# Reordering the lead of a fused attention and feed-forward kernel, with the first unit's variance and the next coarse scores each a slot later

## The chip, the cores and the metric

One core of a Trainium2 chip runs the whole program. The metric is the device time in microseconds. The kernel before took 765.53 us, the median of three runs (765.14 to 766.44). Engine names: PE is TensorE, DVE is VectorE, ACT is ScalarE, POOL is GpSimd, SP is the engine that issues the DMAs.

## The reference

Three layers in a row, over q, k, v of shape (4, 8, 576, 64), batch, heads, positions, head size, all in float32:

```python
# 1. attention: a coarse part on means over 4 positions, and a local part with |i-j| < 4
out_up    = repeat(softmax(q_d @ k_d.T / 8) @ v_d, 4)
out_local = softmax(where(|i-j| < 4, q @ k.T / 8, -1e9)) @ v
x = (out_up + out_local) laid out as (4, 576, 512)
# 2. layer norm and a feed-forward layer, 512 -> 2048 -> 512, with a residual
xn = (x - mean(x)) / sqrt(var(x) + 1e-6) * g_ln
x = x + relu(xn @ w_ch1) @ w_ch2
# 3. token shift, a squared-relu feed-forward layer 512 -> 1024 -> 512 and a gate
xk = mu_k*x + (1-mu_k)*x_prev;  xr = mu_r*x + (1-mu_r)*x_prev
out = sigmoid(xr @ w_r) * (relu(xk @ w_k)**2 @ w_v)
```

## The kernel before

The 2304 rows are cut into 8 units of 288. Attention of a unit is cut again into 3 windows of 96 rows (n = 0, 1, 2) for the local part, and into 2 halves of the heads for the coarse part. Each of the large products is three matmuls, since each float32 operand is split into a "hi" part, rounded to fp32r, and a "lo" part, the rest; ACT makes the hi parts and DVE or POOL the lo parts.

**The lead.** Unit 0's attention comes first, with nothing beside it. Its steps are `Tk`/`Tq` (turn k and q on PE), `Sd`/`S` (coarse and local scores), `PdT`/`PT` (turn the probabilities), `OD`/`AV` (coarse and local values) and `M` (mean for the layer norm). They are listed in `FIRST` (line 66) with the PSUM pair that each uses, and written out by hand in every engine's program (PE: from line 1170 on). `keep_on` (line 938) issues matmuls whose result nobody reads. PE then waits for the centred x of unit 0 (`x_lo`) and starts the feed-forward.

**The blocks.** The feed-forward of layer 2 is a loop over `m` from 0 to 127 (`M_ALL`), 16 blocks for a unit. In block m, PE issues `up_b(m)` (12 matmuls of 288 columns into psH), `attend(2m)`, `down_b(m-1)` (12 matmuls into psY) and `attend(2m+1)`. ACT makes `h_hi(m)` from psH, DVE makes `h_lo(m)`, and `down_b(m)` waits for it (`h_split`).

**The slots.** `attend(slot)` issues the attention steps of the next unit whose slot it is. `LATER` (line 75) gives the slots, 2 for each block; for unit 1 `BEHIND` = 2 is added. So the coarse scores `Sd(1,0)` stand in slot 4, and `S(1,0)` and `Sd(1,1)` in slot 7. `OWN_FIRST` sets the slot of unit 0's variance `V(0)`: 2. What the other engines do for a step follows at a lag from the step's slot: in `ACT_WORK` the exponentials `exp_d` of `Sd` have lag 1; in `DVE_WORK` the maximum `top_d` of `Sd` lag 0 and the sum `sum_d` lag 2; in `POOL_WORK` `norm_d` lag 2, and for `V` `rstd` lag 1. SP stores and loads rstd 3 and 10 slots behind `V`.

**The PSUM pair of the later steps.** All steps of units 1 to 7 use pair 0 (psA). Before a step writes it, `wait_bank_out` (line 450 on) waits until the step before it on that pair has been read out. `S(1,0)` comes next on the pair after `Sd(1,0)`; for an `Sd` the wait is

```python
            elif kind == "Sd":
                eng.wait_ge(d_exped, 2 * u + n + 1)
```

and `d_exped` is raised by the last exponential of `exp_d`. `Sd(1,1)` shares the bank pair with `S(1,0)` and waits for nothing of this kind.

**Order on ACT in a block of unit 0.** It is the order of the text: `h_hi(m)`; then the hi parts of the pieces of w_ch1 that `W1_M` (line 177) gives for block m; then the hi part of one piece of w_ch2, `("w2", (m+1)//4, m+1)`; then `attend(2m)`; `attend(2m+1)`. So block 3 makes the piece `("w2", 1, 4)`, the first of the second quarter of w_ch2, and waits for its load:

```python
                elif name == "w2":
                    act.wait_ge(w2_in[j], 16)
```

**Order on DVE in a block of unit 0.** `h_lo(m)`, `attend(2m)`, the lo parts of the w_ch1 pieces by `W1_M`, `attend(2m+1)`. The weights' quarters are loaded by SP in a fixed order; `load_w2(1)`, the second quarter of w_ch2, is issued behind w_ch1's four. PE's `up_b(4)` needs all four pieces (1, 0) to (1, 3) of w_ch1.

Of the kernel before, what the change touches and what calls it, by code (L numbers as in the profile page):

```python
# [21 lines left out]
def fused_kernel(nc, q, k, v, g_ln, w_ch1, w_ch2, mu_k, mu_r, w_k, w_v, w_r, od_scr, x2_scr, out):  # L22
# [38 lines left out]
    def first_key(w, b):  # L61
# [3 lines left out]

    FIRST = [("Tk", 0, 0, 0), ("Tq", 0, 0, 1), ("G", 0, 0, 3), ("S", 0, 0, 2), ("Tk", 0, 1, 3), ("Tq", 0, 1, 0), ("Tk", 0, 2, 1),
# [3 lines left out]
    N_FIRST = len(FIRST)  # L70

    SLOTS = 2 * NF1
# [12 lines left out]

    OWN = [(0, "V", 0)]

    OWN_FIRST = [(2, "V", 0)]

    ROOT_OUT, ROOT_IN = 3, 10  # L90
    BEHIND = 2
# [3 lines left out]
    KEEP = 256  # L95
# [2 lines left out]

    later = []
    for u in range(1, NU):  # L100
        later += [(SLOTS * (u - 1) + s + (BEHIND if u == 1 else 0), kind, u, n) for s, kind, n in LATER]
    for u in range(NU):
        later += [(SLOTS * u + s, kind, u, n) for s, kind, n in (OWN if u else OWN_FIRST)]
    later.sort(key=lambda x: x[0])
# [65 lines left out]
    for b in range(1, B):  # L170
        behind = BEHIND if b == 1 else 0
        for g, (s, load) in enumerate(((16 + behind, 8), (22, 17 + behind), (28 + behind, 21 + behind), (39, 31))):
# [1 line left out]
            V_LOAD[SLOTS * (2 * b - 2) + load] = (b, g)  # L174


    W1_M = {0: [(1, 0)], 1: [(1, 1)], 2: [(1, 2), (1, 3)], 3: [(2, 0)], 4: [(2, 1)], 5: [(2, 2)],
            6: [(2, 3)], 7: [(3, 0)], 8: [(3, 1)], 9: [(3, 2)], 10: [(3, 3)]}
    M_ALL = NU * NF1
    M_LAST = M_ALL - NF1  # L180
# [14 lines left out]
    with ExitStack() as ctx:  # L195
# [65 lines left out]
        kT = sb(ctx, "kT", [P, KT, S])  # L261
# [9 lines left out]
        ident = sb(ctx, "ident", [P, P])  # L271
# [623 lines left out]
        def _(pe):  # L895
# [29 lines left out]
            def turn_d(u, n):  # L925
                i = place_of["PdT", u, n]
                pe.wait_ge(d_normed, 2 * u + n + 1)
                wait_bank_out(pe, i)
                p = coarse(prob_slot("Sd", u, n), u, n)
                for par in range(2):  # L930
                    for j in range(2):
                        for kh in range(2):
                            at = (2 * j + kh) * GU
                            ins = nc.tensor.transpose(pairs[pair_at(i)][0:GU, par, at:at + GU], p[:, par, j, kh * GU:(kh + 1) * GU],  # L934
                                                      ident[0:GU, 0:GU])
                ins.then_inc(pdt_done, 1)

            def keep_on(n, pair):

                for _ in range(n):  # L940
                    mm(pairs[pair][:, 1, 0:KEEP], ident[:], kT[:, 0, 0:KEEP], start=True, stop=True, skip_group_check=True)

            def add_values():
                for half in range(2):
# [7 lines left out]
            def values_d(u, n):  # L952
                i = place_of["OD", u, n]

                pe.wait_ge(vd_made, 4 * (u // 2) + 2)
                if u == 0 and n == 1:
                    pe.wait_ge(vd_first, 1)
                pe.wait_ge(pdt_out, 2 * u + parts_of("OD", u, n)[-1] + 1)
                wait_bank_out(pe, i)
                for part in parts_of("OD", u, n):  # L960
                    pt = turned_place("PdT", u, part)
                    for j in range(2):
                        for par in range(2):
                            for kh in range(2):
                                at = par * 4 * GU + (2 * j + kh) * GU
                                ins = mm(pairs[pair_at(i)][D * par:D * par + D, 0, (2 * part + j) * GU:(2 * part + j + 1) * GU],  # L966
                                         vd[0:GU, kh, 2 * (2 * part + j) + par, :], pt[0:GU, at:at + GU],
                                         start=(kh == 0), stop=(kh == 1), skip_group_check=True)
                ins.then_inc(od_done, 1)
# [24 lines left out]
            def turn_p(u, n):  # L994
                i = place_of["PT", u, n]
                w = NW_U * u + n
                pe.wait_ge(normed, w + 1)
                wait_bank_out(pe, i)
                p = prob_slot("S", u, n)[0:ROWS]
                for j in range(KT):  # L1000
                    ins = nc.tensor.transpose(turned_bank(i)[:, j * ROWS:(j + 1) * ROWS],  # L1001
                                              p[:, 2 * j * RB:2 * j * RB + RB + KB], ident[0:ROWS, 0:ROWS])
                ins.then_inc(pt_done, 1)

            def values(u, n):
                i = place_of["AV", u, n]
                for part in parts_of("AV", u, n):
                    pe.wait_ge(pt_out, NW_U * u + part + 1)
                    wait_vw(pe, NW_U * u + part)
                wait_bank_out(pe, i)  # L1010
                for part in parts_of("AV", u, n):
                    vw = vw_slot(NW_U * u + part)
                    pt = turned_place("PT", u, part)
                    place = local_place("AV", u, part, BQ)
                    for j in range(KT):
                        for par in range(2):
                            for bl in range(BLOCKS):
                                row = RB * (par ^ bl)
                                keys = slice(row, row + KB)
                                at = j * ROWS + bl * RB  # L1020
                                ins = mm(place[D * par:D * par + D, bl, j], vw[keys, bl, j, :], pt[keys, at:at + BQ],  # L1021
                                         start=True, stop=True, skip_group_check=True)
                ins.then_inc(av_done, 1)
# [160 lines left out]
            add_values()  # L1184
            turn_d(0, 0)
            pe.wait_ge(masked, NW_U)
            keep_on(1, 3)
            turn_d(0, 1)
            values(0, 0)
            pe.wait_ge(vd_first, 1)  # L1190
            keep_on(1, 2)
            turn_p(0, 1)
            values_d(0, 0)
            values_d(0, 1)
            turn_p(0, 2)
            keep_on(1, 2)
            values(0, 1)
            values(0, 2)
            pe.wait_ge(consts, 7)
            keep_on(1, 2)  # L1200
            mean_first(0)
            keep_on(1, 2)
            mean_first(1)
            keep_on(1, 2)
            mean_first(2)
            keep_on(5, 2)
            for slot in range(-LEAD, 0):
                attend(slot)
            for m in range(M_ALL):
# [21 lines left out]
        def _(act):  # L1231
# [54 lines left out]
            def od_o(u, n):  # L1286
                i = place_of["OD", u, n]
                first, last = parts_of("OD", u, n)[0], parts_of("OD", u, n)[-1]
                act.wait_ge(od_done, count_of("OD", u, n))
                if u:  # L1290

                    act.wait_ge(av_done, count_of("AV", u, 0))
                if u >= 1:
                    act.wait_ge(x_made, NW_U * u)
                src = pairs[pair_at(i)][:, 0, 2 * first * GU:2 * (last + 1) * GU]

                nc.scalar.activation(odT[:, 2 * first:2 * (last + 1), :], src.rearrange("p (j g) -> p j g", g=GU), ACT.Copy,
                                     scale=1.0 / FACTOR).then_inc(od_out, 1)
# [140 lines left out]
            pdt_o(0, 1)  # L1439
            pt_o(0, 1)  # L1440
            od_o(0, 0)
            od_o(0, 1)
            pt_o(0, 2)
            hi_weight("w1", 0, 0)
            hi_weight("w1", 0, 1)
            hi_x_first(0)
# [43 lines left out]
        def _(dve):  # L1490
# [264 lines left out]
            for m in range(M_ALL):  # L1755
                u, f = divmod(m, NF1)
                dve.wait_ge(h_hi_ready, m + 1)
                nc.vector.scalar_tensor_tensor(out=h_lo[:, m % 2], in0=psH[:, m % 2, 0:N], scalar=0.0, in1=h_hi[:, m % 2].bitcast(F32),  # L1758
                                               op0=ALU.max, op1=ALU.subtract).then_inc(h_split, 1)
                if m == 0:  # L1760
                    for i in range(HALF):
                        flip("q", 1, 0, i)
                attend(2 * m)
                if m == 1:
                    for i in range(HALF):
                        sum_flipped("q", 1, 0, i)
                if u == 0:
                    for x_ in W1_M.get(f, []):
                        lo_weight("w1", *x_)
                if u == NU - 1:  # L1770
                    if f == 1:
                        dve.wait_ge(av_done, count_by("AV", NU))
                        dve.wait_ge(pt_out, NWIN)
                        nc.vector.memset(x_sh[:, 0, :, 0:1], 0.0).then_inc(lead_zero, 1)
                    if f - 1 in EARLY:
                        lo_mix(0, EARLY[f - 1])
                    if f in EARLY:
                        mix_part(0, EARLY[f])
                    for i in c_weights(f):
                        lo_weight(*c_pieces[i])  # L1780
                if f == 0 and u >= 1:
                    scale_y(u - 1)
                attend(2 * m + 1)
            def lo_k(c, f):
                n = tiles[c][1]
                m = c * NF2 + f
# [64 lines left out]
```

## Time and profile before

| what | value |
|---|---|
| median of 3 runs | 765.53 us |
| the profiled execution | 765.75 us |
| its span | 763.6 us |
| PE busy | 750.5 us, 98% |
| DVE, ACT, POOL busy | 431.5, 272.6, 232.5 us |
| PE in 0 to 10 us | 4.74 us busy |
| PE in 30 to 40 us | 7.86 us busy |
| PE in 50 to 60 us | 10.00 us busy |

The span is the time from the first to the last instruction in the trace; the execution's own time is 2.15 us longer. A timeline row gives the start, the duration, the engine, the line, the output and the inputs, and in brackets how long the engine was idle before it and what ended the idle time. Rows of equal instructions are merged ("x12").

### The profile page before, as it was taken

To read this page: it belongs to the slowest core of one execution; us is meant where nothing else is said; L and a number is where in the kernel's file an instruction comes from. 1 tells how busy PE (TensorE), PEld (TensorE's weight loads), DVE (VectorE), ACT (ScalarE), POOL (GpSimd) and SP (SyncE) were. 2 spreads that over 40 slices of the span, in tenths; PEclk is the share of its full clock that TensorE was granted. 3 is DMA by queue.
4 is the path that set the end of the run, shared out by engine and by line. 5 is a ranking of instruction groups with operands and counts; after the bars stand their busy time and mean duration, and the time that the engine had idled before them with its cause. 6 is when DMAs were issued, how large, how long until landed. Compare 5 with 4: busy or idle time off the path is not lost.

```text
span 763.6 us, 15851 instructions
## 1 busy us (share of the span) xinstructions
PE 750.5 (98%) x6455; PEld 691.8 (91%) x6455; DVE 431.5 (57%) x805; ACT 272.6 (36%) x620; POOL 232.5 (30%) x268
## 2 busy tenths in 40 slices
PE   6899999999999999999999999999999999999998
PEld 5789999999999999999999999998888888888886
DVE  5686863444644354554354332657686776766655
ACT  3854432323223123233223231546334334333322
POOL 4667753132443233345224222004111111111101
PEclk9999999999999999999999999999999999999999
DMA  9894441120450021341011004612003010010010
GB/s 182 209 310 74 93 105 21 27 75 19 86 117 9 16 54 56 71 93 40 14 26 40 15 2 155 215 56 87 0 2 109 1 56 28 1 55 1 1 55 28
DMA packets 116543, 49.67 MB, mean 65 GB/s; under 512 B 95084, under 2 KB 105592, under 8 KB 116472
## 3 DMA queue, kind: packets, MB, share of 16 engines
q1 hardware_dynamic: 116472, 48.68, 25.2%
q8 instruction: 51, 0.84, 0.5%
q14 instruction: 20, 0.16, 0.1%
HBM read 39.20 MB, written 9.45 MB: 64 GB/s over the span
## 4 chain that ended last, share of the span: by engine, by line
PE 94%; SPq 4%; DVE 1%; issue 0%; DMA 0%; ACT 0%; DVEq 0%; ACTq 0%
PE psH L1093 27%; PE psY L1110 27%; PE psH L1144 13%; PE psY L1165 13%; PE psA L1126 6%; PE psA L990 2%; PE psA L1021 2%; SPq L620 1%; PE psA L921 1%; SPq L601 1%; PE psA L966 1%; PE psA L1001 1%; PE psA L934 1%; SPq L589 1%; SPq L624 0%
## 5 line engine op out<-in xcount | busy, mean ns | idle before, releaser
L1093 PE MATMUL psH<-xc_hi,w_hi 128*128 128x288 f32 x512 | 155.0, 303 | 0.5 <-DVE xc_lo L1617 0.5
L1110 PE MATMUL psY<-h_hi,w_hi 128*128 128x288 f32 x512 | 153.0, 299 | 0.0
L1093 PE MATMUL psH<-xc_lo,w_hi 128*128 128x288 f32 x512 | 151.1, 295 | 0.0
L1093 PE MATMUL psH<-xc_hi,w_lo 128*128 128x288 f32 x512 | 151.0, 295 | 0.0
L1110 PE MATMUL psY<-h_lo,w_hi 128*128 128x288 f32 x512 | 150.7, 294 | 0.0
L1110 PE MATMUL psY<-h_hi,w_lo 128*128 128x288 f32 x512 | 150.7, 294 | 0.0
L1758 DVE SCALAR_TENSOR_TENSOR h_lo<-psH,h_hi 128x288 fp32r<-128x288 f32 x128 | 58.3, 456 | 163.3 <-ACT h_hi L1458 162.9
L1458 ACT ACTIVATE h_hi<-psH 128x288 fp32r<-128x288 f32 x128 | 52.4, 410 | 244.4 <-PE psH L1093 243.8
L890 POOL TENSOR_TENSOR relu_k<-relu_k 128x512 f32<-128x512 f32 (+1 forms) x39 | 38.6, 991 | 243.7 <-ACT relu_k L1413 243.7
L1093 PEld LDWEIGHTS psH<-xc_hi,w_hi 128*128 128x128 f32 x512 | 96.1, 188 | 3.5 <-issue 2.2
L1110 PEld LDWEIGHTS psY<-h_hi,w_hi 128*128 128x128 f32 x512 | 96.0, 188 | 1.7 <-issue 1.3
L1093 PEld LDWEIGHTS psH<-xc_hi,w_lo 128*128 128x128 f32 x512 | 96.3, 188 | 0.0
L1110 PEld LDWEIGHTS psY<-h_lo,w_hi 128*128 128x128 f32 x512 | 96.1, 188 | 0.1
L1093 PEld LDWEIGHTS psH<-xc_lo,w_hi 128*128 128x128 f32 x512 | 96.2, 188 | 0.0
L1110 PEld LDWEIGHTS psY<-h_hi,w_lo 128*128 128x128 f32 x512 | 96.0, 188 | 0.0
L1717 DVE RECIPROCAL gate<-gate 128x256 f32<-128x256 f32 x36 | 63.1, 1754 | 1.2
L1165 PE MATMUL psY<-w_hi,kh_hi 128*128 128x512 f32 x144 | 56.3, 391 | 0.2 <-DVE kh_lo L1795 0.2
L1165 PE MATMUL psY<-w_lo,kh_hi 128*128 128x512 f32 x144 | 56.1, 390 | 0.0
L1165 PE MATMUL psY<-w_hi,kh_lo 128*128 128x512 f32 x144 | 56.1, 389 | 0.0
L1413 ACT ACTIVATE relu_k<-psH 128x512 f32<-128x512 f32 (+2 forms) x41 | 22.2, 544 | 59.4 <-PE psH L1144 59.4
L1700 DVE SCALAR_TENSOR_TENSOR mixin<-x_sh,params,mixin 128x512 f32<-128x512 f32 (+1 forms) x40 | 34.8, 871 | 14.5 <-ACT mixin L1383 13.2
L829 POOL TENSOR_TENSOR x<-x,y_tmp 128x288 f32<-128x288 f32 x32 | 25.7, 833 | 48.5 <-DVE y_tmp L1664 48.5
(191 smaller groups left out, 1347.2 us busy)
## 6 DMA issues: line engine op xcount, KB each, us to landing
w_raw<-in_moe_w_ch_dram SPq DMA_DIRECT2D x8, 1024.0 KB, 8.6
v_win<-in_v_dram SPq DMA_DIRECT2D x84, 56.0 KB
x_scratch<-x SPq DMA_DIRECT2D x8, 576.0 KB, 4.5
out_dram<-gate SPq DMA_DIRECT2D x17, 256.0 KB, 2.1
raw<-in_q_dram SPq DMA_DIRECT2D x112, 36.0 KB, 2.1
raw<-in_k_dram SPq DMA_DIRECT2D x96, 36.0 KB, 2.0
v_raw<-in_v_dram SPq DMA_DIRECT2D x12, 288.0 KB
x_sh<-x_scratch SPq DMA_DIRECT2D x3, 1026.0 KB, 5.7
```

Source lines behind the costliest of these rows:

```text
L829: nc.gpsimd.tensor_tensor(x[:, u % 2, d], x[:, u % 2, d], y_tmp[:, d % 2], ALU.add).then_inc(x2_made, 1)
L890: nc.gpsimd.tensor_tensor(r, r, r, ALU.mult).then_inc(k_square, 1)
L1093: ins = mm(psH[:, m % 2, 0:N], ws[a][:, kt, f * P:(f + 1) * P], xx[bb][:, kt], start=(kt == 0 and i == 0), stop=(kt == KT - 1 and i == 2))
L1110: ins = mm(psY[:, d, 0:N], ws[a][:, f, d * P:(d + 1) * P], hs[bb][:, m % 2], start=(f == 0 and i == 0), stop=(f == NF1 - 1 and i == 2))
L1126: ins = mm(psA[:, u % 2, :], xx[a][:, kt, t * P:(t + 1) * P], ws[bb][:, kt, :], start=(kt == 0 and i == 0), stop=(kt == KT - 1 and i == 2))
L1144: ins = mm(psH[:, m % 2, 0:n], ws[a][:, kt, f * P:(f + 1) * P], xx[bb][:, kt, 0:n], start=(kt == 0 and i == 0), stop=(kt == KT - 1 and i = ...
L1165: ins = mm(psY[:, t, :], hs[a][:, m % 2, t * P:(t + 1) * P], ws[bb][:, f, :], start=(f == 0 and i == 0), stop=(f == NF2 - 1 and i == 2))
L1413: nc.scalar.activation(relu_k[:, m % 2, at], psH[:, m % 2, at], ACT.Relu).then_inc(k_relu, 1)
L1458: nc.scalar.activation(h_hi[:, m % 2], psH[:, m % 2, 0:N], ACT.Relu).then_inc(h_hi_ready, 1)
L1700: nc.vector.scalar_tensor_tensor(out=y, in0=x_sh[:, c % 2, kt, 1:n + 1], scalar=(muk_col, mur_col)[which][:, kt:kt + 1], in1=y, op0=ALU.mu ...
L1717: chain(nc.vector.reciprocal(g, g))
L1758: nc.vector.scalar_tensor_tensor(out=h_lo[:, m % 2], in0=psH[:, m % 2, 0:N], scalar=0.0, in1=h_hi[:, m % 2].bitcast(F32), op0=ALU.max, op1 ...
```

## The change

- `FIRST` and PE's hand-written lead: `turn_p(0, 1)` comes ahead of `values(0, 0)`, `turn_p(0, 2)` ahead of `values_d(0, 1)`. `keep_on` takes the columns of one matmul, and stands at other places: 10 of 256 columns and one of 128, where there were 11 of 256. ACT's copies follow the new order: `pt_o(0, 2)` ahead of `od_o(0, 1)`.
- `OWN_FIRST`: `V(0)` goes from slot 2 to slot 3, from ahead of `down_b(0)` to behind it.
- `Sd(1, 0)` goes from slot 4 to slot 5, from ahead of `down_b(1)` to behind it, and all its work on ACT, DVE and POOL goes one slot on with it.
- `W1_M`: the pieces of the second quarter of w_ch1 are made in blocks 1, 2, 2, 3 in place of 0, 1, 2, 2, on ACT (hi) and on DVE (lo), and the order of the weights' semaphore counts follows.
- DVE in block 1: `attend(3)` comes ahead of `sum_flipped("q", 1, 0, i)`.

```diff
--- before.py
+++ after.py
@@ -65,7 +65,7 @@
 
     FIRST = [("Tk", 0, 0, 0), ("Tq", 0, 0, 1), ("G", 0, 0, 3), ("S", 0, 0, 2), ("Tk", 0, 1, 3), ("Tq", 0, 1, 0), ("Tk", 0, 2, 1),
              ("S", 0, 1, 2), ("S", 0, 2, 3), ("Sd", 0, 0, 0), ("Sd", 0, 1, 1), ("PT", 0, 0, 2), ("PdT", 0, 0, 0), ("PdT", 0, 1, 1),
-             ("AV", 0, 0, 3), ("PT", 0, 1, 2), ("OD", 0, 0, 0), ("OD", 0, 1, 1), ("PT", 0, 2, 2), ("AV", 0, 1, 0), ("AV", 0, 2, 1),
+             ("PT", 0, 1, 2), ("AV", 0, 0, 3), ("OD", 0, 0, 0), ("PT", 0, 2, 2), ("OD", 0, 1, 1), ("AV", 0, 1, 0), ("AV", 0, 2, 1),
              ("M", 0, 0, 2), ("M", 0, 1, 3), ("M", 0, 2, 0)]
     N_FIRST = len(FIRST)
 
@@ -85,7 +85,7 @@
 
     OWN = [(0, "V", 0)]
 
-    OWN_FIRST = [(2, "V", 0)]
+    OWN_FIRST = [(3, "V", 0)]
 
     ROOT_OUT, ROOT_IN = 3, 10
     BEHIND = 2
@@ -98,7 +98,7 @@
 
     later = []
     for u in range(1, NU):
-        later += [(SLOTS * (u - 1) + s + (BEHIND if u == 1 else 0), kind, u, n) for s, kind, n in LATER]
+        later += [(SLOTS * (u - 1) + s + (BEHIND + int((kind, n) == ("Sd", 0)) if u == 1 else 0), kind, u, n) for s, kind, n in LATER]
     for u in range(NU):
         later += [(SLOTS * u + s, kind, u, n) for s, kind, n in (OWN if u else OWN_FIRST)]
     later.sort(key=lambda x: x[0])
@@ -174,7 +174,7 @@
             V_LOAD[SLOTS * (2 * b - 2) + load] = (b, g)
 
 
-    W1_M = {0: [(1, 0)], 1: [(1, 1)], 2: [(1, 2), (1, 3)], 3: [(2, 0)], 4: [(2, 1)], 5: [(2, 2)],
+    W1_M = {1: [(1, 0)], 2: [(1, 1), (1, 2)], 3: [(1, 3), (2, 0)], 4: [(2, 1)], 5: [(2, 2)],
             6: [(2, 3)], 7: [(3, 0)], 8: [(3, 1)], 9: [(3, 2)], 10: [(3, 3)]}
     M_ALL = NU * NF1
     M_LAST = M_ALL - NF1
@@ -937,8 +937,7 @@
 
             def keep_on(n, pair):
 
-                for _ in range(n):
-                    mm(pairs[pair][:, 1, 0:KEEP], ident[:], kT[:, 0, 0:KEEP], start=True, stop=True, skip_group_check=True)
+                mm(pairs[pair][:, 1, 0:n], ident[:], kT[:, 0, 0:n], start=True, stop=True, skip_group_check=True)
 
             def add_values():
                 for half in range(2):
@@ -1184,26 +1183,28 @@
             add_values()
             turn_d(0, 0)
             pe.wait_ge(masked, NW_U)
-            keep_on(1, 3)
+            keep_on(KEEP, 3)
             turn_d(0, 1)
+            pe.wait_ge(vd_first, 1)
+            keep_on(KEEP, 2)
+            turn_p(0, 1)
             values(0, 0)
-            pe.wait_ge(vd_first, 1)
-            keep_on(1, 2)
-            turn_p(0, 1)
             values_d(0, 0)
+            keep_on(KEEP // 2, 2)
+            turn_p(0, 2)
             values_d(0, 1)
-            turn_p(0, 2)
-            keep_on(1, 2)
             values(0, 1)
+            keep_on(KEEP, 2)
             values(0, 2)
             pe.wait_ge(consts, 7)
-            keep_on(1, 2)
+            keep_on(KEEP, 2)
             mean_first(0)
-            keep_on(1, 2)
+            keep_on(KEEP, 2)
             mean_first(1)
-            keep_on(1, 2)
+            keep_on(KEEP, 2)
             mean_first(2)
-            keep_on(5, 2)
+            for _ in range(4):
+                keep_on(KEEP, 2)
             for slot in range(-LEAD, 0):
                 attend(slot)
             for m in range(M_ALL):
@@ -1439,8 +1440,8 @@
             pdt_o(0, 1)
             pt_o(0, 1)
             od_o(0, 0)
+            pt_o(0, 2)
             od_o(0, 1)
-            pt_o(0, 2)
             hi_weight("w1", 0, 0)
             hi_weight("w1", 0, 1)
             hi_x_first(0)
@@ -1762,6 +1763,7 @@
                         flip("q", 1, 0, i)
                 attend(2 * m)
                 if m == 1:
+                    attend(2 * m + 1)
                     for i in range(HALF):
                         sum_flipped("q", 1, 0, i)
                 if u == 0:
@@ -1780,7 +1782,8 @@
                         lo_weight(*c_pieces[i])
                 if f == 0 and u >= 1:
                     scale_y(u - 1)
-                attend(2 * m + 1)
+                if m != 1:
+                    attend(2 * m + 1)
             def lo_k(c, f):
                 n = tiles[c][1]
                 m = c * NF2 + f
```

## Rows read from the trace of the kernel before

**Rows 1.** The page's first part: busy time, share of the span, instructions.
```profile
PE 750.5 (98%) x6455; PEld 691.8 (91%) x6455; DVE 431.5 (57%) x805; ACT 272.6 (36%) x620; POOL 232.5 (30%) x268
```
**Rows 2.** Waits of PE: line, releaser, total us, times, longest us.
```profile
PE psA L905 <- POOL masks L770: 4.8, 1, 4.8
PE psA L1050 <- POOL xs L818: 1.4, 1, 1.4
...
PE psA L921 <- DVE qdT L1500: 0.5, 1, 0.5
```
**Rows 3.** Chain of waits, 0 to 100 us: start, us, what.
```profile
44.30 1.80 PE psY L1110 x12
46.11 1.60 PE psH L1093 x12
47.70 1.58 PE psY L1110 x12
```
**Rows 4.** Timeline of PE around blocks 1 to 5.
```profile
39.16 0.72 PE L1050 MATMUL psA<-xs,ones 128*128 128x288 f32 x2 [1.45 <-POOL xs L818]
...
43.59 0.71 PE L921 MATMUL psA<-kdT,qdT 64*72 64x144 f32 x8 [0.55 <-DVE qdT L1500]
...
49.22 0.68 PE L990 MATMUL psA<-kT,qT 64*64 64x56 f32 x32
49.83 0.71 PE L921 MATMUL psA<-kdT,qdT 64*72 64x144 f32 x8
50.47 0.40 PE L1093 MATMUL psH<-xc_hi,w_hi 128*128 128x288 f32 x1
...
55.49 0.67 PE L934 MATMUL psA<-ident,prob 72*72 72x72 f32 x8
```
**Rows 5.** Timeline of ACT in blocks 2 to 4.
```profile
45.45 0.38 ACT L1255 ACTIVATE prob<-psA,bias_d 72x144 f32<-72x144 f32 x1 [0.23 <-DVE bias_d L1531]
...
46.80 0.20 ACT L1255 ACTIVATION_READ_ACCUMULATOR prob<-psA,bias_d 72x1 f32 x1
47.74 0.41 ACT L1458 ACTIVATE h_hi<-psH 128x288 fp32r<-128x288 f32 x1 [0.74 <-PE psH L1093]
48.05 0.72 ACT L1338 ACTIVATE w_hi<-w_raw,params 128x512 fp32r<-128x512 f32 x1
51.60 0.62 ACT L1352 CAST w_hi<-w_raw 128x512 fp32r<-128x512 f32 x1 [2.83 <-DMA w_raw<-in_moe_w_ch_dram]
52.38 0.41 ACT L1458 ACTIVATE h_hi<-psH 128x288 fp32r<-128x288 f32 x1 [0.16 <-PE psH L1093]
...
53.30 0.61 ACT L1352 CAST w_hi<-w_raw 128x512 fp32r<-128x512 f32 x1
53.80 0.37 ACT L1255 ACTIVATE prob<-psA,bias_d 72x144 f32<-72x144 f32 x1
```
**Rows 6.** The DMA issues, timeline of SP.
```profile
39.04 0.65 SPq L624 DMA_DIRECT2D w_raw<-in_moe_w_ch_dram  x1
...
42.13 3.05 SPq L633 DMA_DIRECT2D w_raw<-in_moe_w_ch_dram  x3
```
**Rows 7.** DMA view of 38 to 52 us: mean rate of the window.
```profile
DMA packets 3836, 4.36 MB, mean 312 GB/s; under 512 B 1937, under 2 KB 1937, under 8 KB 3833
```
**Rows 8.** Timeline of PE in the lead.
```profile
12.34 1.54 PE L905 MATMUL psH<-ident,k_first 96*128 96x96 f32 x8 [0.67 <-DMA k_first<-in_k_dram]
13.81 1.97 PE L990 MATMUL psY<-kT,qT 64*64 64x56 f32 x64
15.76 1.24 PE L921 MATMUL psA<-kdT,qdT 64*72 64x144 f32 x8
16.79 0.71 PE L921 MATMUL psH<-kdT,qdT 64*72 64x144 f32 x8
```
**Rows 9.** ACT, then DVE and POOL at the lead's end, timelines.
```profile
26.92 0.29 ACT L1297 ACTIVATE odT<-psH 128x144 f32<-128x144 f32 x1 [0.21 <-PE psH L966]
27.31 0.62 DVE L1589 TENSOR_TENSOR x<-psY,odT 128x192 f32<-128x192 f32 x2 [3.92 <-ACT odT L1297]
29.24 0.59 POOL L811 TENSOR_TENSOR xs<-x 128x192 f32<-128x192 f32 x1 [0.17 <-DVE x L1589]
```
**Rows 10.** DVE and POOL around the next unit's scores, timelines.
```profile
50.65 0.62 DVE L1556 TENSOR_TENSOR prob<-psA,masks 112x448 f32<-112x448 f32 x1 [1.09 <-PE psA L990]
...
52.62 1.01 DVE L1531 TENSOR_SCALAR bias_d<-top_d 72x4 f32<-72x4 f32 x1
...
56.65 1.15 POOL L787 TENSOR_TENSOR prob<-prob,inv_d 72x576 f32<-72x576 f32 x1
```

## The prediction

> **What bounds the kernel now.** I read the page's first part, then PE's waits, then the timelines of the stretch that the change touches. PE is busy for 750.5 of 763.6 us [rows 1], so only two things count: time in which PE stands still, and the rate at which it runs. The change touches two of PE's waits: 1.4 us ahead of the variance (L1050, for POOL's sum of squares) and 0.5 us ahead of the next coarse scores (L921, for the group sums of q) [rows 2]. They look like the prize, about 2 us. What remains is PE's own work, 1.6 us for each product of 12 matmuls [rows 3], and everybody else runs in its shadow. So the question at every moved step is whether it now stands behind something that arrives late.
>
> **One thing arrives late: the second quarter of w_ch2.** In block 3 ACT stands still for 2.83 us before the cast at 51.60, and a load of weights ends that wait [rows 5]. SP issued this load in the group at 42.13, behind a quarter of w_ch1 at 39.04 and another just before it [rows 6]. The DMA moved 4.36 MB in 38 to 52 us [rows 7], and three quarters of 1 MB each plus the value windows are about what had to pass before it. Nothing in the change touches SP's order or its waits there (only the store and the load of rstd go one slot on, long behind these loads). So I take the landing at 51.55 as fixed on the clock, wherever PE is. In the kernel before it costs PE nothing: all that stood behind the cast on ACT was `h_hi` of block 4, which ran at 52.38 and had itself waited only 0.16 us, for PE [rows 5].
>
> **Coarse scores a slot later: the step that decides.** `exp_d(1,0)` has lag 1. With `Sd(1,0)` in slot 4 it belongs to slot 5, the end of block 2 on ACT: it ran at 45.45 and ended at 47.00 (46.80 + 0.20), ahead of `h_hi(3)` at 47.74 [rows 5]. With `Sd(1,0)` in slot 5 it belongs to slot 6. That is block 3, and there ACT issues it behind the weights, so behind the cast at 51.60. PE's `S(1,0)` in slot 7 writes the PSUM pair that `Sd(1,0)` filled, and waits for `d_exped`, the end of these exponentials. `S(1,0)` ran at 49.22 without a wait [rows 4]. Now it comes as follows:
> - the cast starts at 51.60, and the next ACT instruction starts 0.50 us behind the start of such a cast (53.30 to 53.80) [rows 5]: exponentials from 52.10;
> - they take 1.55 us as a set (45.45 to 47.00) [rows 5]: end at 53.65;
> - I add 0.1 us, an estimate, for the semaphore: `S(1,0)` at 53.75.
>
> That is 53.75 − 49.22 = 4.53 us later than before. Behind it on PE stand `Sd(1,1)`, `up_b(4)` and all the rest, and no other work can pass. From there each engine's work hangs on PE's progress as before, so the 4.5 us stay to the end.
>
> **The slot's other work.** `sum_d(1,0)` on DVE goes to slot 7, where it stands behind the mask of `S(1,0)` and `top_d(1,1)`; `norm_d(1,0)` on POOL stands behind `sub(1,0)`. The turn `PdT(1,0)` needs it 6.27 us behind the start of `S(1,0)` (49.22 to 55.49) [rows 4]. The mask started 1.43 us behind that start, and `bias_d`, after which `sum_d` can come, ended 4.41 us behind it (52.62 + 1.01) [rows 10]. The sum and its reciprocal need some 0.35, `norm_d` 1.15 [rows 10]: 5.9 us, 0.4 ahead of the need. I cost it at nothing; if POOL's pass is as slow as its neighbours under contention, 0.4 us more.
>
> **The variance behind `down_b(0)`.** The 1.45 us wait [rows 4] goes: 1.6 us of product [rows 3] now stand where PE waited, and POOL's sum ends at about the same moment as that product. `Sd(1,0)` comes behind `down_b(1)` and loses its 0.55 us [rows 4]. `h_lo(1)` on DVE comes earlier, since no piece of weights stands before it in block 0. So PE reaches the end of `down_b(2)` about 2.0 us earlier: before, that end was at about 49.2 (47.70 + 1.58) [rows 3], now about 47.2. All of this gain is lost: PE only arrives earlier at a wait whose end is set by the DMA.
>
> **The pieces of w_ch1 a block later.** `up_b(4)` needs the piece (1,3), which ACT now makes in block 3, ahead of the late cast, at about 46 us, and DVE straight behind it. Needed at 55. Free by 7 us, because the stall covers it; without the stall it would be free by about 1 us. The piece costs 0.72 us on ACT [rows 5], wherever it stands.
>
> **The lead.** `od_o(0,1)` on ACT goes behind `pt_o(0,2)`, from 26.92 to about 27.7, and the first `x_o` on DVE waits for it: from 27.31 to about 28.05 [rows 9]. POOL's second partial sum at 29.24 [rows 9] moves too, by about 0.6, and a `keep_on` now stands ahead of the last local values. Against that the other values come some 0.2 earlier. I expect the feed-forward to start 0 to 0.6 us later, and this too vanishes in the wait for the DMA, as would any shift smaller than about 6 us. Half a `keep_on` less is about 0.25 us, equally covered.
>
> **The rate of PE after the stall.** PE stands still from about 47.2 to 53.75, 6.5 us (6 with a later lead). Before, the longest pause after 5 us was 1.45 us [rows 4], and the rate held. At the start it was otherwise: after 4.8 us without work [rows 2], the 8 coarse matmuls took 1.24 us at 15.76, and the same 8 took 0.71 at 16.79 [rows 8]. The granted clock reads 1.00, the 2.4 GHz level, over all of that, so only the durations show it. The engine had run without a pause since 12.34 when it rose, 4.4 us. A pause of 6.5 us is nearer to the 4.8 than to the 1.45, so I expect the slow rate again behind the stall. The bounds: 0 if the rate holds; and if it stays slow as long as in the lead, from 4.84 to 16.8, 12 us times 0.43 (1 − 0.71/1.24) is 5.1 us. I take the 4.4 us of unbroken work, as what follows the stall is unbroken as well: 4.4 times 0.43 is 1.9 us.
>
> The Trainium skill ("TensorE: Matmul & The Clock Gate", "HAM oscillation — how this bites in real kernels") says that a wait for data in which the array idles too long puts its clock back to half, and that the work behind it starts cold each time. By it the loss is sure and the sum is the one with the 1.9; if the granted clock of the profile is right in never falling, the sum is the one without.
>
> **Sum.** Span 763.6 + 4.5 + 1.9 = 770.0; with 2.15 us around the span 772.2; the profiled execution is 0.2 above the median of the runs, so 772.0.
>
> **Rivals.**
> - *The stall with no loss of rate.* For it: the granted clock reads 1.00 everywhere. Against: the two durations of [rows 8]. 765.5 + 4.5 = 770.0.
> - *The stall with a long slow stretch, or a second wait* (`PdT(1,0)` on `norm_d`). 765.5 + 4.5 + 5.1 = 775.1 at the far end, 773.5 to 775 in all. For it: the lead's slow stretch. Against: that was small matmuls with pauses, and behind the stall stand full products.
> - *Faster: the load lands in time.* One mechanism: the second quarter of w_ch2 in SBUF when ACT reaches its cast at about 46.9. Then nothing holds `exp_d(1,0)`, and what counts is the gain of 2.0 us less a lead later by up to 0.6: 765.5 − 1.6 = 763.9. It would need a landing 4.5 us earlier than the 51.55 of the trace. Break-even is a landing near 47.1. Against it: 4.36 MB in 14 us [rows 7], with the DMA full. For it: only that one execution was profiled.
> - *The change doesn't do what it says.* If ACT's order let the exponentials pass the cast, that is the same 763.9. The text puts them behind.
>
> **Chances.** The forecast (stall and a slow stretch of ordinary length) 0.55, with 771 to 773.5 as its own range; stall at full rate 0.23; stall with more 0.12; faster 0.07; load just in time, so that gain and loss cancel, 0.03. A measurement of this kernel can tell about 0.2% from no change, 1.5 us. Slower by more than that: 0.55 + 0.23 + 0.12 = 0.90; within 0.03; faster 0.07. The range 769.4 to 774.6 leaves out the faster case, the cancelling one and the upper tail of the long slow stretch.
>
> **What would show it.** In the profile after: a wait of PE of about 6 us at L990 on psA, with ACT's L1255 as its releaser, which isn't there before; on ACT the order cast (L1352) at about 51.6 after some 5 us idle, then four exponentials; the waits at L1050 and L921 gone or below 0.3 us; `Sd(1,1)` at 1.1 to 1.3 us for its 8 matmuls in place of 0.71, and the products behind it at up to twice 1.6 us for some 4 us; no new wait behind 60 us. I am wrong if the cast comes much before 51 us, if `S(1,0)` starts before 52, or if PE's L990 waits for something else.

## The result

The changed kernel takes 771.35 us (median of 12 runs, 767.48 to 772.40); the kernel before took 765.39 in the same rounds. The ratio is 1.0059, 95% interval 1.0041 to 1.0078: slower by 6.0 us in the medians. The ratio takes every execution in, and two of the 12 of the kernel before took 769.5 and 770.0 us; by the medians alone it would be 1.0078. The forecast was 772.0, range 769.4 to 774.6.

The execution that was profiled is the fastest of the 12, 767.48 us with a span of 764.9, so its trace shows the mechanism at its mildest. The page's first part, which answers to [rows 1]:

```profile
PE 752.1 (98%) x6455; PEld 693.7 (91%) x6455; DVE 429.2 (56%) x805; ACT 272.6 (36%) x620; POOL 232.2 (30%) x268
```

As many matmuls as before, one of them shorter by 128 columns, and PE is busy for 1.6 us more: that is a slower rate, not more work. A second execution of the same kernel was profiled too (769.60 us, span 767.1; experiment 11). PE's waits, first trace and then second (line, releaser, total us, times, longest):

```profile
PE psA L905 <- DMA k_first<-in_k_dram: 4.7, 1, 4.7
PE psA L989 <- ACT prob L1256: 2.2, 1, 2.2
PE psH L1092 <- DVE xc_lo L1618: 1.0, 1, 1.0
```
```profile
PE psA L989 <- ACT prob L1256: 4.0, 1, 4.0
```

The two waits of [rows 2] at L1050 and L921 are gone, and a new one stands at `S(1,0)` (L989), released by the exponentials, as the forecast said. The timeline of PE in the first trace, which answers to [rows 4]:

```profile
38.89 0.72 PE L1049 MATMUL psA<-xs,ones 128*128 128x288 f32 x2
...
42.74 0.71 PE L921 MATMUL psA<-kdT,qdT 64*72 64x144 f32 x8
...
46.53 0.29 PE L1109 MATMUL psY<-h_hi,w_lo 128*128 128x288 f32 x1
49.01 0.68 PE L989 MATMUL psA<-kT,qT 64*64 64x56 f32 x32 [2.19 <-ACT prob L1256]
49.62 0.71 PE L921 MATMUL psA<-kdT,qdT 64*72 64x144 f32 x8
...
50.50 0.29 PE L1092 MATMUL psH<-xc_lo,w_hi 128*128 128x288 f32 x1
50.63 0.34 PE L1092 MATMUL psH<-xc_hi,w_lo 128*128 128x288 f32 x1
50.77 0.44 PE L1092 MATMUL psH<-xc_hi,w_hi 128*128 128x288 f32 x1
```

The variance and the coarse scores run without a wait, and `down_b(2)` is through at 46.8 us (46.53 + 0.29), 2.5 us earlier than before; 0.3 of that is a feed-forward that starts earlier in this execution (33.91 against 34.21). Then PE stands still. `S(1,0)` starts at 49.01, 0.2 earlier than the 49.22 of before, so in this execution the pause itself cost nothing net. What cost is the last row: from 50.77 on each product matmul takes 0.44 in place of 0.29 us. `PdT(1,0)` starts at 56.68, 1.19 later than before [rows 4], and the span is 1.3 longer. The clock is in the windows (us, busy of PE, PEld, DVE, ACT, POOL, granted clock, DMA share, GB/s):

```profile
50.00:51.00 1.00, 1.00 (x10) 0.81 (x7) 0.56 (x1) 0.00 (x0) 0.00 (x0) 0.87 1.05 365
51.00:52.00 1.00, 1.00 (x6) 1.00 (x6) 0.97 (x3) 0.00 (x0) 0.20 (x1) 0.50 1.46 210
```

0.50 is the 1.2 GHz level. It lasted from 50.7 to about 54.1.

ACT shows why the two traces differ. In the first, the four pieces of weights run without a gap and the exponentials start at 47.32; in the second the cast waits for its load:

```profile
45.28 0.41 ACT L1459 ACTIVATE h_hi<-psH 128x288 fp32r<-128x288 f32 x1 [1.89 <-PE psH L1092]
45.59 1.32 ACT L1339 ACTIVATE w_hi<-w_raw,params 128x512 fp32r<-128x512 f32 x2
46.81 0.60 ACT L1353 CAST w_hi<-w_raw 128x512 fp32r<-128x512 f32 x1
47.32 0.37 ACT L1256 ACTIVATE prob<-psA,bias_d 72x144 f32<-72x144 f32 x1
```
```profile
48.90 0.62 ACT L1353 CAST w_hi<-w_raw 128x512 fp32r<-128x512 f32 x1 [1.70 <-DMA w_raw<-in_moe_w_ch_dram]
49.42 0.37 ACT L1256 ACTIVATE prob<-psA,bias_d 72x144 f32<-72x144 f32 x1
```

In the second trace `S(1,0)` starts at 51.11 and `PdT(1,0)` at 58.91: 1.9 us of delay and 1.5 us of slow rate, 3.5 us of span. So the same program sees this load land by 46.8 in one execution and at 48.9 in another; in the kernel before it was 51.6 [rows 5]. Most of that comes from when SP issues it, 38.20 and 39.54 here (first trace, then second) against 42.13 [rows 6]:

```profile
38.20 2.61 SPq L633 DMA_DIRECT2D w_raw<-in_moe_w_ch_dram  x3
```
```profile
39.54 3.83 SPq L633 DMA_DIRECT2D w_raw<-in_moe_w_ch_dram  x3
```

From this issue to the start of the cast there are 9.4 us in the second trace and 9.5 in the kernel before.

### The profile page after: what moved, and what is told of

Its sections match the earlier page's. It is cut to its first block, busy times and chain, and to the rows that moved or that the text cites. A ratio compares the mean times of both kernels' runs of the same rounds, so it can differ in the third digit from the quotient of the medians.

```text
span 764.9 us, 15851 instructions
## 1 busy us (share of the span) xinstructions
PE 752.1 (98%) x6455; PEld 693.7 (91%) x6455; DVE 429.2 (56%) x805; ACT 272.6 (36%) x620; POOL 232.2 (30%) x268
## 4 chain that ended last, share of the span: by engine, by line
PE 96%; DVE 2%; ACT 1%; issue 1%; DMA 0%; POOL 0%; DVEq 0%; SPq 0%; ACTq 0%
PE psH L1092 27%; PE psY L1109 27%; PE psH L1143 13%; PE psY L1164 13%; PE psA L1125 6%; PE psA L1020 2%; PE psA L989 2%; PE psA L921 1%; PE psA L965 1%; PE psA L1000 1%; PE psA L934 1%; DMA k_first<-in_k_dram 0%; PE psA L905 0%; DVE xc_lo L1618 0%; PE psA L1025 0%
```

## The experiments

Every kernel ran beside the kernel before, which took 765.1 to 765.4 us (medians) in the rounds. Ratios are to it, over all executions. Of the diffs the lines that differ are shown, some of them cut short. Kernel 1 is the kernel of experiment 1, and so on.

**1. Sd(1,0) back in slot 4, all else as changed.**

```diff
-(BEHIND + int((kind, n) == ("Sd", 0)) if u == 1 else 0)
+(BEHIND if u == 1 else 0)
```

> The changed kernel with the next coarse scores Sd(1,0) back in slot 4, all else as changed. My theory (the loss is the exponentials of Sd(1,0) behind the weight casts of block 3 on ACT, and PE's S(1,0) behind them): the wait of 2 to 6 us at S(1,0) and the slow stretch behind it are gone. PE then waits up to 1.5 us for the group sums of q ahead of Sd(1,0) instead. Median 763.5 to 765.5, against 771.35 for the change, and a spread of under 1.5 us. Rival (the loss lies in the variance's place, the weights a block later or the lead): the time stays near 771.

767.19 us, ratio 1.0022 [1.0003, 1.0041]. The wait at `S(1,0)` is gone and one of 1.4 us at `Sd(1,0)` has come, as expected. But the runs fall in two groups: 6 of 12 at 765.0 to 765.7, 6 at 768.7 to 770.1. The first lies at the upper end of what I expected, the second outside it, and so do the median and the spread. The second group was a puzzle, taken up in 7 to 9.

**2. The exponentials first in block 3.** In block 3 ACT issues `attend(6)` ahead of the weights, else as changed.

```diff
+                if m == 3:
+                    attend(2 * m)
                 if u == 0:
                     for x_ in W1_M.get(f, []):
...
-                attend(2 * m)
+                if m != 3:
+                    attend(2 * m)
```

> The changed kernel, but in block 3 ACT issues attend(6), the exponentials of Sd(1,0), ahead of the weights' hi parts. My theory: S(1,0) starts 0.5 us or less behind down_b(2), near 47.3 us, the pause and the slow stretch are gone, median 763 to 764.5, below the kernel before, since the two waits that the change removes are then really removed. Rival 1 (PE would wait for something else there, such as the piece (1,3) of w_ch1 or the second quarter of w_ch2): a new wait of 1 to 4 us at up_b(4) or down_b(4), median 766 to 769. Rival 2 (the slot of Sd is innocent): 771.

764.92 us, ratio 0.9989 [0.9970, 1.0009], 6.4 us below the change with nothing but ACT's order altered. Every other part of the change is in this kernel, so none of them makes the loss by itself. I had expected 763 to 764.5; that it is faster than the kernel before isn't shown, since the interval takes in 1. `S(1,0)` starts at 47.70, 0.4 later than I expected. The wait that remains there is 1.0 us: 0.44 of it because the maximum on DVE stands behind two weight pieces, the rest the exponentials themselves:

```profile
47.70 0.68 PE L989 MATMUL psA<-kT,qT 64*64 64x56 f32 x32 [1.00 <-ACT prob L1256]
```

**3. The kernel before with only Sd(1,0) in slot 5.** The diff of 1, the other way round.

> The kernel before with only Sd(1,0) moved from slot 4 to 5. My theory: this alone makes the loss. S(1,0) starts at 50.4 if the second quarter of w_ch2 has landed early (as in the profiled execution of the change) and at 53.7 if it lands at 51.6, so 1.2 to 4.5 us later than before, plus 0 to 2 us of slow rate: median 767 to 772, with a spread over 2 us. Rival (the slot move is harmless by itself, the loss needs the other parts): 765 to 765.8, spread under 1.5 us.

771.46 us, ratio 1.0074 [1.0053, 1.0096]; 6 runs of 771.13 to 771.88. The moved slot alone makes as much as the whole loss. I was wrong on the spread: under 1 us. The trace has both causes, first ACT, then PE, then the windows:

```profile
49.57 0.62 ACT L1352 CAST w_hi<-w_raw 128x512 fp32r<-128x512 f32 x1 [2.34 <-DMA w_raw<-in_moe_w_ch_dram]
...
51.44 0.20 ACT L1255 ACTIVATION_READ_ACCUMULATOR prob<-psA,bias_d 72x1 f32 x1
```
```profile
51.78 1.11 PE L990 MATMUL psA<-kT,qT 64*64 64x56 f32 x32 [4.03 <-ACT prob L1255]
52.83 1.24 PE L921 MATMUL psA<-kdT,qdT 64*72 64x144 f32 x8
...
60.61 0.66 PE L934 MATMUL psA<-ident,prob 72*72 72x72 f32 x8
```
```profile
50.00:55.00 5.00, 3.22 (x44) 2.77 (x45) 0.80 (x2) 1.64 (x9) 1.26 (x1) 0.60 1.03 311
55.00:60.00 5.00, 5.00 (x30) 5.00 (x29) 2.90 (x7) 2.72 (x10) 3.20 (x3) 0.71 0.36 57
```

`S(1,0)` is 2.56 us later than before (behind a pause of 4.03 us), and from it to `PdT(1,0)` there are 8.83 us, where there were 6.27 [rows 4]: 2.56 of delay and 2.56 of slow rate, together 5.1 of the 5.2 us of span. The coarse scores take 1.24 us here, as in the lead [rows 8], this time with a granted clock that shows it.

**4. The pause filled.** As changed, with 12 matmuls of 256 columns between `down_b(2)` and `S(1,0)`; nobody reads what they write.

```diff
+                if m == 3:
+                    for _ in range(12):
+                        mm(psH[:, 0, 0:KEEP], ident[:], kT[:, 0, 0:KEEP], start=True, stop=True, skip_group_check=True)
```

> The changed kernel with 12 extra matmuls of 256 columns, about 5.6 us, on PE between down_b(2) and S(1,0), that is in the pause; their result is not read. Theory A (the pause also lowers the rate of PE behind it, which costs 1.5 to 2.5 us): no stretch behind S(1,0) with a granted clock below 1.00; in executions with a late load the pause was 6 us anyway, so the median falls from 771.35 to 768.5 to 770. Theory B (the rate costs nothing of note; the loss is the pause alone): the median stays at 771 to 772, and where the load lands early it is 3 us above what it was.

769.65 us (768.71 to 770.52), ratio 1.0046 [1.0026, 1.0066]. With 5.34 us of useless work the median is 1.7 us below that of the change; the two sets overlap (767.48 to 772.40 there) and so do the intervals, so what is firm is that the work costs nothing. In the trace the granted clock stays at 1.00 (the row shows 24 for the 12, two records for each):

```profile
46.91 5.34 PE L1217 MATMUL psH<-kT,ident 128*128 128x256 f32 x24
52.18 0.68 PE L989 MATMUL psA<-kT,qT 64*64 64x56 f32 x32
```
```profile
50.00:55.00 5.00, 5.00 (x62) 4.21 (x61) 1.35 (x3) 0.00 (x0) 0.03 (x1) 1.00 0.80 189
```

`S(1,0)` is 2.96 us later than before and the span 3.0 longer: with the rate kept, the later start costs its own length and no more.

**5. The load earlier.** As changed, the second quarter of w_ch2 issued ahead of window 4 and w_ch1's last quarter.

```diff
+            load_w2(1)
             load_window(4)
             load_w1(3)
-            for j in range(1, 4):
+            for j in range(2, 4):
```

> The changed kernel with one edit on SP: the load of the second quarter of w_ch2 is issued ahead of the value window 4 and the last quarter of w_ch1, so that it lands some 3 us earlier. Theory (two causes in series hold the exponentials: the landing of that load in most executions, and where it is early, ACT's own work in block 3, 0.4 + 1.2 + 0.5 us behind up_b(3)): the pause ahead of S(1,0) falls to about 2.2 us in most executions, and the median from 771.35 to 767 to 769, with the lowest run unchanged at about 767.5. Rival (the landing doesn't matter, ACT's order alone does): the median stays at 771 with the same spread.

767.39 us (765.89 to 768.70), ratio 1.0009 [0.9989, 1.0028]. So 4.0 of the 6.0 us hang on when this load lands. In its trace the wait at `S(1,0)` is 2.2 us, and ACT's cast (at 47.20) does not wait for the load: ACT's own work in block 3 holds the rest.

```profile
49.40 0.98 PE L990 MATMUL psA<-kT,qT 64*64 64x56 f32 x32 [2.19 <-ACT prob L1257]
50.31 1.24 PE L922 MATMUL psA<-kdT,qdT 64*72 64x144 f32 x8
```

`PdT(1,0)` starts at 57.17, 7.77 us behind `S(1,0)`, so the slow rate costs 1.50 us here. I was wrong on the lowest run, which I took to stay at 767.5: four of the 12 take 765.9 to 766.3 at a mean clock of 1.000, the other eight 767.4 to 768.7 at 0.995 to 0.998. By that the rate fell in most of these executions and not in all; no trace of one of the four was taken.

**6. The exponentials in block 2.** As changed, but ACT issues `exp_d(1,0)` at slot 5, and DVE makes its maximum ahead of block 2's two weight pieces.

```diff
+                 if s + lag - int((kind, u, n, what) == ("Sd", 1, 0, "exp_d")) == slot]
...
+                if m == 2:
+                    attend(2 * m + 1)
                 if u == 0:
                     for x_ in W1_M.get(f, []):
                         lo_weight("w1", *x_)
```

> The changed kernel with the coarse scores left in slot 5, but ACT issues their exponentials at the end of block 2 (slot 5, as before the change), and DVE makes their maximum at slot 5 ahead of the two weight pieces of block 2. Theory: S(1,0) then starts at 46.7 with no wait, 1.0 us earlier than with the exponentials first in block 3 (764.92), so 763.5 to 764.3, and no slow stretch. Rival (h_hi(3) now comes 1 us later on ACT, or the pieces of weights on DVE, and PE waits for them at up_b(4) instead): 764.5 to 766.

764.33 us, ratio 0.9981 [0.9961, 1.0000]. `S(1,0)` starts at 46.91 with no wait. (DVE leaves out the `attend` at the end of block 2 in return.)

**7. Sd(1,0) in slot 4, its wait filled.** Kernel 1 with three `keep_on(KEEP, 0)` ahead of `attend(4)` in block 2.

> The changed kernel with Sd(1,0) back in slot 4, and 3 extra matmuls of 256 columns, about 1.3 us, in the wait of 1.4 us ahead of it. With Sd(1,0) in slot 4 and no extra matmuls 6 of 12 executions took 765.0 to 765.7 us at a mean granted clock of 1.000, and 6 took 768.7 to 770.1 at 0.996 to 0.998. Theory (a pause of 1.4 us is enough to lower the rate in about half the executions): the second group is gone, all runs 765 to 766. Rival (the second group comes from the load of the weights or the lead): it stays in a quarter to a half of the runs.

765.78 us, ratio 1.0004 [0.9979, 1.0029], but 5 of 12 runs stay at 768.1 to 769.9. The theory fell: the 1.4 us pause doesn't make the second group. The execution in the trace is of the first group (765.02 us).

**8. Kernel 1 once more.**

> The kernel with Sd(1,0) back in slot 4 once more, for a look: half of its executions took 768.7 to 770.1. If this one does, the trace shows the wait; theory: a late landing of weights holds ACT in block 3 or 4 and PE behind it, 1 to 3 us, with a slow stretch behind. Rival: no wait, but a stretch of the lead or of block 2 at the lower clock. If it takes 765, it tells nothing.

773.30 us, and it told two things, neither as expected. First, `PdT(1,0)` waits 2.0 us for the exponentials of `Sd(1,1)`, with no late load. Second, the clock was at its lower level in the lead: granted 0.50 from 25 to 30 us and 0.67 in 35 to 40, with the same 8 turns that took 0.69 us before at 1.16. It fell right behind a wait of 1.05 us: 
```profile
21.13 1.16 PE L934 MATMUL psA<-ident,prob_first 72*72 72x72 f32 x8 [1.05 <-POOL prob_first L787]
...
62.72 0.67 PE L934 MATMUL psA<-ident,prob 72*72 72x72 f32 x8 [2.03 <-ACT prob L1256]
```
```profile
25.00:30.00 5.00, 5.00 (x67) 4.20 (x66) 0.00 (x0) 1.18 (x3) 0.00 (x0) 0.50 0.96 234
```

Two to nine of the runs of the kernel before in each set (770 us at a mean clock of 0.991 to 0.993, against 765 at 1.000) look like this second thing; I have no trace of one.

**9. Kernel 1 with the load earlier.** The diff of 5 on kernel 1.

> The kernel with Sd(1,0) back in slot 4 (6 of 12 executions at 765, 6 at 769) and the second quarter of w_ch2 loaded ahead of window 4 and of w_ch1's last quarter. Theory (the slow half is a late landing of that load): all executions 765 to 766. Rival (it is the lead, the clock after the wait of 1.4 us, or another load): a quarter to a half stay at 768 to 770.

768.77 us, ratio 1.0042 [1.0029, 1.0054]; the 5 runs lie at 767.0 to 769.1. The theory fell the other way round: an earlier load puts its executions in the second group. PE, DVE and POOL in its trace, and below them DVE and POOL of the first trace of kernel 1 (765.59 us):

```profile
56.65 1.11 PE L935 MATMUL psA<-ident,prob 72*72 72x72 f32 x8 [2.03 <-ACT prob L1257]
...
47.92 3.52 DVE L1653 SCALAR_TENSOR_TENSOR w_lo<-w_raw,params,w_hi 128x512 fp32r<-128x512 f32 x2
51.36 0.61 DVE L1558 TENSOR_TENSOR prob<-psA,masks 112x448 f32<-112x448 f32 x1
...
48.08 1.56 POOL L788 TENSOR_TENSOR prob<-prob,inv_d 72x576 f32<-72x576 f32 x1 [3.29 <-DVE inv_d L1543]
49.61 1.28 POOL L836 TENSOR_TENSOR w_lo<-w_raw,w_hi 128x512 fp32r<-128x512 f32 x1
```
```profile
48.49 2.27 DVE L1652 SCALAR_TENSOR_TENSOR w_lo<-w_raw,params,w_hi 128x512 fp32r<-128x512 f32 x2
...
48.65 1.56 POOL L787 TENSOR_TENSOR prob<-prob,inv_d 72x576 f32<-72x576 f32 x1 [3.27 <-DVE inv_d L1542]
50.41 1.52 POOL L835 TENSOR_TENSOR w_lo<-w_raw,w_hi 128x512 fp32r<-128x512 f32 x1 [0.19 <-ACT w_hi L1353]
```

With the change's later pieces, DVE makes two of them in block 3 beside POOL's `norm_d(1,0)`. The first piece starts ahead of `norm_d` and takes 0.72 us; `norm_d` takes 1.56, where it takes 1.14 in the trace of the change. The second piece, begun under `norm_d`, takes 2.88 us here and in the trace of experiment 8, where DVE stays out over two POOL instructions, and 1.63 in the first trace of kernel 1. The later mask, maximum and exponentials then make `PdT(1,0)` 2 us late. The clock falls behind that pause here (0.67 over 55 to 60 us), and did not in experiment 8; of the 5 runs two take 767.0 and 767.8 at a mean clock of 1.000, three 768.8 to 769.1 at 0.998.

The gap of 0.19 us between POOL's two instructions isn't what decides. The trace of experiment 7 shows no such gap, and DVE's second piece takes 1.63 us there too, while POOL's piece takes 1.74 in place of 1.28:

```profile
47.81 2.27 DVE L1655 SCALAR_TENSOR_TENSOR w_lo<-w_raw,params,w_hi 128x512 fp32r<-128x512 f32 x2
...
47.97 1.56 POOL L787 TENSOR_TENSOR prob<-prob,inv_d 72x576 f32<-72x576 f32 x1 [3.28 <-DVE inv_d L1545]
49.50 1.74 POOL L835 TENSOR_TENSOR w_lo<-w_raw,w_hi 128x512 fp32r<-128x512 f32 x1
```

What parts the four traces is when ACT's cast for POOL's piece ends. Where DVE lost, it ended 0.7 us ahead of the end of `norm_d` (48.97 against 49.64, 55.04 against 55.72); where DVE got in, 0.1 ahead or 0.1 behind (49.42 against 49.53, 50.33 against 50.22). So an earlier load makes the late case likelier. This is read from four traces; no experiment moved one of these instructions alone.

The Trainium skill ("SBUF — State Buffer", "Who interferes with whom") calls the ports that the two engines share an exclusive lock, for which a VectorE instruction with two SBUF inputs contends with a GpSimd instruction that reads SBUF. The rows agree, with 2.88 us in place of 0.72. In the change itself this doesn't happen, since with `Sd(1,0)` in slot 5 `norm_d` comes later than these pieces (53.10 in the first trace).

**10. The lead alone.** The kernel before with the change's lead on PE and ACT.

> The kernel before with the lead's part of the change alone: PE's new order and keep_on, ACT's new order. The traces suggest that this part costs: from turn_d(0,0) to the first up_b there are 11.96 us before and 12.58 with the change. Theory: 0.3 to 0.6 us slower than before, 765.7 to 766.0. Rival (the lead gains, as the values' turn comes earlier): 764.8 to 765.2.

765.96 us against 765.36, ratio 1.0003 [0.9987, 1.0018]: not resolved by the runs. In the trace the distance from `turn_d(0,0)` to the first `up_b` is 21.42 to 34.00, so 12.58 us, the same as with the whole change (21.33 to 33.91) and 0.62 more than before (22.25 to 34.21). That is what the medians differ by too (0.6).

**11. The change once more.**

> The changed kernel once more, for a second look at its trace: 11 of its 12 executions took 1.4 to 5 us longer than the profiled one, in which the load had landed before ACT asked for it. Theory: in an ordinary execution the cast of the second quarter's first piece waits for its load, S(1,0) starts at 51 to 54 us, behind a pause of 4 to 6.5 us, and the slow stretch lies behind it; total 770 to 772. Rival (the longer executions differ elsewhere): S(1,0) at 49 as in the first trace, and the difference at another place.

769.60 us, a little under the 770 to 772 that I expected; shown with the result. The pause was 4.0 us and `S(1,0)` came at 51.11, both at the lower end of what I expected.

**12. What they point to.** Kernel 6 with the lead of before and the load of 5.

> What the experiments point to: the variance behind down_b(0) and the scores in slot 5 as in the change, exponentials on ACT in slot 5, their maximum on DVE ahead of block 2's weights (764.33 with the change's lead), the lead as it was before the change (its new order cost 0.6), and the second quarter of w_ch2 loaded ahead of window 4 and of w_ch1's last quarter. Theory: the parts add, 763.6 to 764.0, with no execution above 766. Rival (the lead's 0.6 is covered by something else now, or the moved load makes w_ch1's last quarter late for block 7): 764.3 to 766.

763.59 us, ratio 0.9976 [0.9955, 0.9996]: faster than both kernels, 1.5 us below the kernel before (765.13 beside it) and 7.8 below the change. Ten runs lie at 762.9 to 764.0, one at 768.5 with a mean clock of 0.991, where I had expected none above 766. The page's first lines, which answer to [rows 1], and PE at `S(1,0)`:

```profile
span 761.0 us, 15851 instructions
...
PE 749.8 (99%) x6455; PEld 691.4 (91%) x6455; DVE 431.1 (57%) x805; ACT 272.5 (36%) x620; POOL 231.2 (30%) x268
```
```profile
46.43 0.68 PE L992 MATMUL psA<-kT,qT 64*64 64x56 f32 x32
```

## Why the prediction was right, step by step

**The step that decides: right.** The exponentials of `Sd(1,0)` went behind the weight casts of block 3 on ACT, and PE's `S(1,0)` behind them. Shown from both sides: the slot move alone gives 771.46, and the change without ACT's order gives 764.92.

**The size of the pause: too large by about 1 us, as far as the runs tell.** I took the landing at 51.55 as fixed, since the change leaves SP's order as it was. That step didn't hold. Other traces with the same SP order have this load in place by 46.8, or at 47.5, 48.8, 48.9, 49.6, 49.7 and 50.7 us (starts of the cast). In the seven in which ACT waited for it, the kernel before among them, the cast starts 8.7 to 9.5 us behind SP's issue; the issue itself lies between 38.2 and 42.1. Why SP gets there earlier in one execution than in another isn't shown. `S(1,0)` was forecast at 53.75 and traced at 49.01 and 51.11 in the change, and at 51.78 in experiment 3. So two of the signs that I had named for being wrong came true, the cast much before 51 us (46.8 and 48.9) and `S(1,0)` before 52, and the wait at L989 was 2.2 and 4.0 us, not about 6. They speak against the fixed landing; the path stands by experiments 2 and 3. The late load is worth 4.0 us (experiment 5).

**The rate behind the pause: right in kind, forecast 1.9, too small by about 0.7 in a median run.** Measured from `S(1,0)` to `PdT(1,0)`, less 6.27: 1.40, 1.53, 2.56 and 1.50 us in the four traces with a pause of 2.2 to 4.0 us (the change twice, experiments 3 and 5), 0.02 with the pause filled. My argument that the granted clock can't show it was wrong: it reads 0.50 here. It reads 1.00 in the first 16 us, where the same matmuls are as slow, for another reason: the trace's record of the clock starts at 16.90 us in the kernel before, with a rise to 1.00, and ahead of it there is nothing to read. I also reasoned that 6.5 us of standing still is near the 4.8 of the start. The rate fell after 2.2 us as well, and not in the execution of experiment 2 that paused for 1.0; but in experiment 8 it fell behind 1.05 us, and in experiment 10 it did not behind the same 1.05. The length of the pause alone doesn't decide it. The Trainium skill ("TensorE: Matmul & The Clock Gate", "HAM oscillation — how this bites in real kernels") has the work behind such a wait start cold. The four traces agree that the clock falls to 0.50; that the work starts cold holds in experiment 3 alone, and in the other three the clock fell 0.2 to 1.7 us after PE was back.

**The sum: right, in part by luck.** No trace of a median run of the change was taken, but the mean clock of every run is known. Eight of the 12 runs of the change, 770.95 to 772.40 us, have 0.995 or 0.996, like the trace of experiment 3 (0.995, 771.26 us), where the lower level lasted 6.8 us and cost 2.56. The two traces of the change have 0.997 and 0.998 and 3.4 us at the lower level. So I estimate that the 6.0 us of the median are some 2.6 of slow rate and 3.4 of delay, against 1.9 and 4.53 in the forecast: one term too small, the other too large, and the errors nearly cancel.

**The two removed waits: right.** Both are gone, and PE is at the end of `down_b(2)` at 46.8 and 47.1 (forecast 47.2). The feed-forward started at 34.21 in the second trace, as before, and there the gain is 2.2 us (forecast 2.0). The gain was lost at the next wait, as forecast; freed in experiment 6, it gives about 1 us.

**The lead: right at its upper end.** 0.62 us longer, forecast 0 to 0.6. Measured from `turn_d(0,0)`, the second coarse copy on ACT (`od_o(0,1)`) starts 0.85 us later and the first `x_o` on DVE 0.86.

**The second wait, on `norm_d`: costed at nothing, and nothing in the change.** `PdT(1,0)` didn't wait in its traces.

**The rival "faster": wrongly built.** I wrote that with the load in place nothing holds the exponentials. But `h_hi(3)` starts at 45.28 in the first trace, released by PE, and to it and what stands behind it go 0.3 us of its own, 1.2 of w_ch1 pieces, 0.5 of the cast and 1.55 of exponentials. So `S(1,0)` comes near 49.0 in the change, load or no load, as late as before, and 763.9 was out of reach. The first trace has the load in place and still takes 767.48. I estimate the right price for an early landing at 765 to 767: no gain, and 0 or 1.4 us for the rate.

## What to carry to other kernels

When a step moves by one slot, follow its work on every engine to the place in that engine's queue: here one slot on ACT meant from ahead of a DMA wait to behind it, in a kernel where that wait had been free. Check then who waits for the read-out of the bank. Price a pause of TensorE with the slow stretch behind it: 1.4 to 2.6 us here, behind pauses of 2.2 to 4.0. And when a wait ends on a DMA, one trace gives one landing; look up when it was issued, and how far that moves between executions, before calling it fixed.

## What the runs showed of the hardware

- The clock can fall late: in the first trace the pause of 2.19 us ended at 49.01, PE then worked for 1.7 us at full rate, and from 50.77 on the matmuls took 0.44 in place of 0.29 us. In experiment 5 a pause of the same 2.19 us was followed by the fall after 0.2 us, and in experiment 3, after 4.03 us, the clock was down when the work came back.
- Useless matmuls in a pause cost nothing here: with 5.34 us of them the median was 1.7 us lower, with overlapping runs, and the clock stayed at 1.00.
- VectorE's 512-column piece takes 0.72 us when it starts ahead of POOL's instruction, 1.63 when it has to let one pass, and 2.88 when it has to let two pass. An earlier load went with a slower kernel in this way (experiment 9).
